# The first products of the MLP moved into the attention's last pair, on one core

## What is computed

```
attention (4 x 8 heads, 576 positions, head size 64):
  scores = q @ k.T / 8
  scores below (row maximum - tau) are dropped; softmax; attn @ v
MLP:      x = attention's output, as [2304, 512]
  h = x @ w_in            # [2304, 2048]
  y = relu(h)**2 @ w_out  # [2304, 512]
experts:  logits = y @ w_gate, best of 8 experts for each token,
  out = gate * sigmoid(y @ w_output_gate)[expert] * (relu(y @ w1[e]) @ w2[e])
```

## Time and profile before

| | us |
|---|---|
| median of 3 runs | 1022.42 |
| lowest and highest | 1020.78, 1023.05 |
| profiled execution, its own time | 1021.32 |
| span of its profile | 1019.6 |
| mean granted TensorE clock | 0.998 |

### The profile page before, as it was taken

The page is one execution under the profiler, slowest core; times in us unless marked ns, Lnnn a source line. Parts: engine busy times, 40 slices in busy tenths (PEclk is TensorE's granted clock), DMA queues, the critical chain, the costliest instruction groups (busy, mean ns, idle before and its releaser), DMA issues.

```text
span 1019.6 us, 19281 instructions
## 1 busy us (share of the span) xinstructions
PE 994.8 (98%) x6731; PEld 828.7 (81%) x6731; DVE 627.0 (61%) x1220; ACT 585.8 (57%) x922; POOL 418.3 (41%) x725
## 2 busy tenths in 40 slices
PE   7999999999998999999999999999999999999996
PEld 5888888888886888888888888889978888888884
DVE  5888888888885334322322232235787777777773
ACT  4888787787774333322322232233548888888883
POOL 4777778778783000000000000000008866666763
PEclk9999999999999999999999999999999999999999
DMA  4322322322213110010011001005389157351110
GB/s 115 80 61 71 86 55 71 87 61 69 59 30 95 42 52 1 21 42 21 1 42 42 0 21 42 22 1 161 124 328 401 49 196 283 116 197 41 34 41 34
DMA packets 85385, 84.04 MB, mean 82 GB/s; under 512 B 49711, under 2 KB 64559, under 8 KB 85298
## 3 DMA queue, kind: packets, MB, share of 16 engines
q1 hardware_dynamic: 81778, 72.41, 23.9%
q0 software_dynamic: 3520, 10.49, 3.0%
HBM read 69.24 MB, written 15.21 MB: 83 GB/s over the span
## 4 chain that ended last, share of the span: by engine, by line
PE 66%; DVE 1%; SPq 0%; issue 0%; ACT 0%; DMA 0%; POOL 0%; ACTq 0%; POOLq 0%; DVEq 0%
PE y_ps L1167 19%; PE h_ps L1150 19%; PE y_ps L1231 16%; PE row_ps L1231 8%; PE h_ps L1262 2%; PE row_ps L1136 2%; PE y_ps L1221 1%; SPq L969 0%; SPq L965 0%; DMA y_rows<-r_buf 0%; DVE g_lo L1488 0%; ACT r_buf L1335 0%; PE h_ps L1136 0%; POOL out_dram L1058 0%; DVE y_row L1701 0%
## 5 line engine op out<-in xcount | busy, mean ns | idle before, releaser
L1483 DVE TENSOR_TENSOR g_buf<-r_buf 128x512 f32<-128x512 f32 (+1 forms) x80 | 51.1, 638 | 220.5 <-ACT r_buf L1335 219.8
L1335 ACT ACTIVATE r_buf<-h_ps 128x512 f32<-128x512 f32 (+1 forms) x80 | 44.4, 555 | 234.1 <-PE h_ps L1150 231.9
L951 POOL TENSOR_TENSOR w_lo<-w_experts,w_hi 128x2048 fp32r<-128x2048 f32 x20 | 126.2, 6309 | 73.9 <-ACT w_hi L1394 73.7
L1394 ACT ACTIVATE w_hi<-w_experts 128x2048 fp32r (+1 forms) x100 | 150.4, 1564 | 0.5 <-PE row_ps L1231 0.5
L1069 POOL MEMSET ones<- 128x128 bf16 x1 | 0.2, 210 | 356.9 <-DVE x_lo L1469 356.9
L477 ACT ACTIVATE e_sb<-s_sb,stats,live 128x576 f32<-128x576 f32 x144 | 124.5, 865 | 37.8 <-POOL stats L265 36.5
L951 DVE TENSOR_TENSOR w_lo<-w_experts,w_hi 128x1024 fp32r<-128x1024 f32 (+1 forms) x80 | 137.0, 1754 | 5.3 <-ACT w_hi L1394 5.0
L1150 PE MATMUL h_ps<-x_hi,w_in_hi 128*128 128x512 f32 (+1 forms) x320 | 119.9, 375 | 2.3 <-DVE x_lo L1469 2.3
L1167 PE MATMUL y_ps<-g_hi,w_out_hi 128*128 128x512 f32 (+1 forms) x320 | 118.0, 369 | 0.9 <-DVE g_lo L1488 0.9
L1150 PE MATMUL h_ps<-x_hi,w_in_lo 128*128 128x512 f32 (+1 forms) x320 | 117.9, 368 | 0.0
L1150 PE MATMUL h_ps<-x_lo,w_in_hi 128*128 128x512 f32 (+1 forms) x320 | 117.8, 368 | 0.0
(11 more groups left out here) (251 smaller groups left out, 2217.8 us busy)
## 6 DMA issues: line engine op xcount, KB each, us to landing
w_experts<-in_moe_w_dram SPq DMA_DIRECT2D x18, 2048.0 KB, 13.9
y_rows<-y_row SPq DMA_DIRECT2D x36, 128.0 KB, 2.4
k_raw<-in_k_dram SPq DMA_DIRECT2D x32, 128.0 KB, 3.1
q_raw<-in_q_dram SPq DMA_DIRECT2D x32, 128.0 KB, 2.9
w_raw<-in_moe_w_in_dram SPq DMA_DIRECT2D x16, 256.0 KB, 3.2
v_nat<-in_v_dram SPq DMA_DIRECT2D x16, 256.0 KB, 2.6
y_T<-in_moe_w_out_dram SPq DMA_DIRECT2D x16, 256.0 KB, 2.7
y_early<-y_row SPq DMA_DIRECT2D x32, 128.0 KB, 2.4
```

The costliest lines, as they stand in the source:

```text
L951: alu.tensor_tensor(group_of(w_lo, g)[:, c0:c1], raw_group(buf, g)[:, c0:c1], group_of(w_hi, g)[:, c0:c1].bitcast(F32), ALU.subtract).then ...
L1394: nc.scalar.activation(group_of(w_hi, g)[:, c0:c1], raw_group(buf, g)[:, c0:c1], ACT.Copy).then_inc(hi_done, 1)
L1483: V.tensor_tensor(g_buf[:, 0:cols], r_buf[:, 0:cols], r_buf[:, 0:cols], ALU.mult).then_inc(sq_done, 1)
```

## The change

It does five things.

1. `x_hi`, `x_lo` and `y_T` get fixed places at the top of SBUF (`con[...]`), and the attention's buffers of the even pairs are allocated last, so that they lie in part under these. `h_ps`, the PSUM tile of the hidden products, is now allocated for both blocks, and the attention uses it as `s_ps[0]`.
2. Splitting the first 512 tokens of x moves into the attention: `first_x_hi(kc)` is the last thing that ACT does in steps 0 to 3 of pair 15, `first_x_lo(kc)` the last thing that DVE does in steps 1 to 4. They write into the places of the even pairs' buffers, so the first waits for the scores of pair 14.
3. The first four w_out loads are issued by SP in the attention once pair 14 is done, and so is the row of zeros, now from `w_raw`, with its memset on POOL ahead of the last `add_eps`. The relu's wait for the zeros is gone; SP waits for them ahead of the end of the block.
4. `first_hidden()`: PE makes the 12 matmuls of `hidden_group(0, 0)` at the end of the attention's block, behind `output_tail(15)`, and waits for their end.
5. In `moe`, `hidden_group(0, 0)` only counts up its semaphore; `split_x_group(0)`, the first loads and the memset are gone.

```diff
 @block.sync (attention), behind the loop over pairs
+            sp.wait_ge(tail_set, PAIRS - 1)
+            for n in range(4):
+                sp.dma_start(w_out_raw[:, n, :], w_out[n * P:(n + 1) * P, :]).then_inc(w_out_in, 16)
+            sp.wait_ge(zero_set, 1)
+            sp.dma_start(y_rows[DUMMY:DUMMY + 1, :], w_raw[0:1, :]).then_inc(zero_out, 16)
+            sp.wait_ge(w_out_in, 64)
+            sp.wait_ge(zero_out, 16)
 @block.gpsimd (attention), at the end
+            pool.wait_ge(w_split, 2 * LAST * PAIRS)
+            V.memset(w_raw[0:1, :], 0.0).then_inc(zero_set, 1)
             add_eps(PAIRS - 1)
 @block.tensor (attention), called behind the loop over steps
+            def first_hidden():
+                pe.wait_ge(xh_done, KC)
+                pe.wait_ge(max_done, CHUNKS * PAIRS)
+                for part, (w, x) in enumerate(((con["w_in_hi"], x_hi), (con["w_in_lo"], x_hi), (con["w_in_hi"], x_lo))):
+                    if part == 2:
+                        pe.wait_ge(xl_done, KC)
+                    for kc in range(KC):
+                        last = pe.matmul(s_ps[0][:, 0, :], w[:, 0, kc, :], x[:, kc * GROUP_T:(kc + 1) * GROUP_T],
+                                         start=(part == 0 and kc == 0), stop=(part == 2 and kc == KC - 1))
+                last.then_inc(hidden_made, 1)
+                pe.wait_ge(hidden_made, 1)
 @block.scalar (attention)
+            def first_x_hi(kc):
+                act.wait_ge(x_main_done, KC)
+                act.wait_ge(scores_ready, CHUNKS * (PAIRS - 1))
+                nc.scalar.activation(x_hi[:, kc * GROUP_T:(kc + 1) * GROUP_T], x_T[:, kc, 0:GROUP_T], ACT.Copy).then_inc(xh_done, 1)
                 if i < PAIRS and len(heads_in(c)) == 2:
                     exponential(i, c, 1)
+                if i == PAIRS - 1 and c < KC:
+                    first_x_hi(c)
 @block.vector (attention)
+            def first_x_lo(kc):
+                dve.wait_ge(xh_done, kc + 1)
+                V.tensor_tensor(x_lo[:, kc * GROUP_T:(kc + 1) * GROUP_T], x_T[:, kc, 0:GROUP_T],
+                                x_hi[:, kc * GROUP_T:(kc + 1) * GROUP_T].bitcast(F32), ALU.subtract).then_inc(xl_done, 1)
                 if c == 3 and i + 1 < PAIRS:
                     ends_lo(i + 1)
+                if i == PAIRS - 1 and 1 <= c <= KC:
+                    first_x_lo(c - 1)
 @block.sync (moe)
-            for n in range(4):
-                sp.dma_start(y_T[:, n, :], w_out[n * P:(n + 1) * P, :]).then_inc(w_raw_in[n], 16)
...
-            sp.wait_ge(zero_set, 1)
-            sp.dma_start(y_rows[DUMMY:DUMMY + 1, :], r_buf[0:1, :]).then_inc(zero_out, 16)
-            sp.wait_ge(zero_out, 16)
 @block.gpsimd (moe)
-            nc.gpsimd.memset(r_buf[0:1, :], 0.0).then_inc(zero_set, 1)
 @block.tensor (moe), hidden_group
+                if n == 0:
+                    pe.sem_inc(h_done, 1)
+                    return
 @block.scalar (moe)
             def split_w_out(f):
-                act.wait_ge(w_raw_in[f % 4], 16 * (f // 4 + 1))
+                if f >= 4:
+                    act.wait_ge(w_raw_in[f % 4], 16 * (f // 4))
...
-                if n == 0:
-                    act.wait_ge(zero_out, 16)
-                else:
+                if n >= 1:
                     act.wait_ge(sq_done, n)
                     act.wait_ge(g_hi_done, n)
...
-            split_x_group(0)
 @block.vector (moe)
-            split_x_group(0)
```

More of the change, by code:

```diff
@@ L98, in sets_in, with attention @@
     return 3 if c < LAST else 2
-def attention(nc, q, k, v, tau, w_in, con):
+def attention(nc, q, k, v, tau, w_in, w_out, y_rows, con):
     ident, x_T = con["ident"], con["x_T"]
+    x_hi, x_lo, w_out_raw = con["x_hi"], con["x_lo"], con["y_T"]
     qf = q.rearrange("b h s d -> (b h) s d")
@@ L116, in sem @@
             return ctx.enter_context(nc.semaphore(name))
-        q_raw = [sb(f"q_raw{b}", [P, QC, P]) for b in range(2)]
-        k_raw = [sb(f"k_raw{b}", [P, QC, P]) for b in range(2)]
-        v_nat = [sb(f"v_nat{b}", [P, 2, QC, D]) for b in range(2)]
+        q_raw, k_raw, v_nat = [None, sb("q_raw1", [P, QC, P])], [None, sb("k_raw1", [P, QC, P])], [None, sb("v_nat1", [P, 2, QC, D])]
         v_odd = [sb(f"v_odd{b}", [P, LAST, D]) for b in range(2)]
         v_mix = [sb(f"v_mix{b}", [P, P]) for b in range(2)]
-        qT_hi, qT_lo = ([sb(f"{n}{b}", [P, QC * P], F32R) for b in range(2)] for n in ("qT_hi", "qT_lo"))
-        kT_hi, kT_lo = ([sb(f"{n}{b}", [P, S], F32R) for b in range(2)] for n in ("kT_hi", "kT_lo"))
+        qT_hi, qT_lo = ([None, sb(f"{n}1", [P, QC * P], F32R)] for n in ("qT_hi", "qT_lo"))
+        kT_hi, kT_lo = ([None, sb(f"{n}1", [P, S], F32R)] for n in ("kT_hi", "kT_lo"))
         s_sb = [[sb(f"s_sb{b}{h}", [P, S]) for h in range(2)] for b in range(2)]
@@ L143, in attention @@
         w_raw = sb("w_raw", [P, WPART])
-        s_ps = [psum(f"s_ps{p}", [P, 2, 512]) for p in range(2)]
+        kept_to = nc.sbuf_base
+        v_nat[0] = sb("v_nat0", [P, 2, QC, D])
+        kT_hi[0], kT_lo[0] = (sb(f"{n}0", [P, S], F32R) for n in ("kT_hi", "kT_lo"))
+        qT_hi[0], qT_lo[0] = (sb(f"{n}0", [P, QC * P], F32R) for n in ("qT_hi", "qT_lo"))
+        q_raw[0], k_raw[0] = sb("q_raw0", [P, QC, P]), sb("k_raw0", [P, QC, P])
+        assert kept_to <= con["y_T_at"]
+        s_ps = [con["h_ps"], psum("s_ps1", [P, 2, 512])]
         t_ps = [psum(f"t_ps{p}", [P, 512]) for p in range(2)]
@@ L179, in attention @@
         x_tail_done = sem("x_tail_done")
+        w_out_in = sem("w_out_in")
+        hidden_made = sem("hidden_made")
+        zero_set, zero_out = sem("zero_row_set"), sem("zero_out")
+        xh_done, xl_done = sem("first_xh_done"), sem("first_xl_done")
         WPIECE = WPART // LAST
@@ L456, in _ @@
                     scores(*divmod(step + 1, STEPS))
+            first_hidden()
         @block.scalar
@@ L701, in moe @@
         w_out_lo = sb("w_out_lo", [P, FC, DM], F32R)
[L702 to L705, removed]
+        x_hi, x_hi_at, x_lo, x_lo_at = con["x_hi"], con["x_hi_at"], con["x_lo"], con["x_lo_at"]
         r_at = nc.sbuf_base
@@ L713, in moe @@
         g_lo = sb("g_lo", [P, 2 * GROUP_T], F32R)
-        y_T_at = nc.sbuf_base
-        y_T = sb("y_T", [P, KC, GROUP_T], F32)
+        y_T, y_T_at = con["y_T"], con["y_T_at"]
         y_row = con["y_row"]
         marks = sb("marks", [P, KC // 2, P + 4 * E], F32)
+        assert nc.sbuf_base <= y_T_at
         def region(at, size):
@@ L780, in moe @@
         factor_parts = on_g_top("factor_parts", [P, COLS, 3], BF16)
-        h_ps = psum("h_ps", [P, 2, 512])
+        h_ps = con["h_ps"]
         y_ps = [psum(f"y_ps{d}", [P, 512]) for d in range(KC)]
@@ L880, in split_before @@
         def split_before(q, kc):
-            return sum(KC * len(pieces(p)) for p in range(q)) + kc * len(pieces(q))
+            return sum(KC * len(pieces(p)) for p in range(1, q)) + kc * len(pieces(q))
         X_READ = split_before(ENDQ, KC)
@@ L1144, in hidden_group @@
                 for kc in range(KC):
-                    if f == 0:
+                    if f == 0 and q >= 1:
                         pe.wait_ge(xh_done, split_before(q, kc + 1))
@@ L1789, in program @@
         con["free_at"] = nc.sbuf_base
-        attention(nc, q, k, v, tau, w_in, con)
+        con["h_ps"] = keep.enter_context(nc.psum_tensor("h_ps", [P, 2, 512], F32))
+        top = nc.sbuf_top
+        for name, shape, dt in (("x_lo", [P, KC * GROUP_T], F32R), ("x_hi", [P, KC * GROUP_T], F32R),
+                                ("y_T", [P, KC, GROUP_T], F32)):
+            top -= 4 * KC * GROUP_T
+            con[name + "_at"] = top
+            con[name] = nc.alloc_sbuf_tensor_at(name, shape, dt, offset=top)
+        attention(nc, q, k, v, tau, w_in, w_out, y_rows, con)
         moe(nc, w_out, w_gate, w_output_gate, w1, w2, y_rows, y_early, out, con)
```

2 lines of the change are left out of this document (removed).

## The result

| | us |
|---|---|
| changed kernel, median of 5 runs | 1030.03 (1028.38 to 1031.66) |
| kernel before, median of 5 runs | 1021.59 (1020.78 to 1023.05) |
| ratio, 95% interval | 1.0077 (1.0065 to 1.0088) |
| profiled execution after: span | 1028.2 (before 1019.6) |

The forecast was 1020.9 with a range of 1019.0 to 1022.5. The page of the changed kernel looks like the page of before, but for one number: PE has the same 6731 matmuls and is busy 9.5 us longer.

The account below looks back on a forecast made before the run. PE, busy 98% of the span, was taken as the bound. A 2.6 us gain at the border less 1.1 for held POOL gave -1.5 us on the profiled 1021.32; against the runs' median the forecast was 1020.9, range 1019.0 to 1022.5.

Parts of the forecast that it names:

- The rest of the kernel shifts as a whole: Beyond the border, MLP and experts keep their pace, as PE is the bound and its progress releases all loads.
- The border: Between attention and MLP, the first output product comes at 323.1 instead of 325.69, a gain of 2.6 us.
- my bound of 2.3: Lowest gain at the border, if PE's wait for its last matmul and the step cost twice 0.31 us.
- The holds: In pair 15, DVE's x_lo subtractions stop POOL's small operations; attention ends 1.1 us later, bounds 0 and 2.8.
- ACT's four copies, the DMAs and the memset: In the attention's end, covered by idle time and so free; uncovered, copies 0.55 us each, memset half a us.
- If the granted clock at the border falls from 1.00, all of part 1 is wrong: Sign set for the border: a clock below 1.00 there would refute its gain and the whole forecast.
- part 1: The gain between attention and MLP from earlier first products, x split and relu: 2.6 us, bounds 2.3 and 3.2.
- C: Rival: DVE becomes the last pair's bound, attention ends 3.7 us later, 1.1 slower in sum, 1023.5; chance 0.06.
- the mark that I had set for it: Sign for the rival of DVE as bound: output_tail ends past 319.6, where the forecast had near 318.2.

Follow-up runs that it names:

- e2: Changed kernel with x_hi, x_lo and y_T 1408 bytes lower, aligned with the other operands as before the change: 1022.13 us, ratio 0.9995.
- e1: Kernel before with only x_hi, x_lo and y_T at the changed kernel's addresses, no work moved: 1030.19 us, ratio 1.0069.
- e5: e4 without first_hidden, so the first 12 products stay in the MLP's block: 1018.46 us, ratio 0.9971.
- e3: Changed kernel with the four x_lo subtractions behind the last reciprocal, in DVE's idle time: 1027.37 us, ratio 1.0043.
- e4: Changed kernel with the three tiles 1408 bytes lower and the x_lo subtractions in DVE's idle time: 1018.85 us, ratio 0.996.
- s2: e4 with x_hi, x_lo, y_T and marks 128 bytes higher: 1027.18 us, a single run.
- s4: e3 with the tiles 128 bytes lower, 1280 bytes off the other operands: 1018.69 us, a single run.
- s1: e4 with x_hi, x_lo, y_T and marks 32 bytes higher: 1029.24 us, a single run.
- s5: e4 with x_hi, x_lo, y_T and marks 64 bytes higher: 1027.84 us, a single run.
- f1: e4 with POOL's last w_in split moved behind the biases and cuts of the last step: 1017.45 us, ratio 0.996.

## Why the prediction was wrong

1. **The step that failed: "The rest of the kernel shifts as a whole".** Item 1 of the change, the new addresses, got no price at all, not even bounds; I read it as what made room for the rest. In its place the runs show that both the MLP and the experts run slower, 232.8 ns for a hidden product instead of 227.4, because three tiles lie 1408 bytes off: 7.9 us (changed kernel to e2, and e1 to the kernel before). No row of before prices a distance directly, but there may have been a trace in it: the hidden products behind the rows at L1136 are slower than others on the same code. A question of it ("why do equal matmuls differ?") would have shown that the pace depends on more than columns and clock.

The Trainium skill would not have warned (page "SBUF — State Buffer", section "Who interferes with whom"): it has PE never waiting on anyone at SBUF. That rule is on one engine against another; the runs show a price without another engine, 227.4 against 232.8 ns by nothing but the distance between PE's own two operands, and the measurement decides.

2. **The border (right in kind, 2.6 forecast, 2.05 found).** The chain was as described: the relu starts right behind its w_out copy (323.90), and its two halves are there at 326.05, 0.35 ahead of PE's own 326.40. The sum is below my bound of 2.3, since PE's pause between the blocks was 0.73, longer than the twice 0.31 that this bound allowed.

3. **The holds (right in kind, 1.1 forecast, 1.66 found for the `biases` of the last step).** I followed POOL's queue up to the second mask and overlooked that x_lo(3) stands on DVE right behind it, so that the same instruction is held twice: 311.04 instead of 310.5. The two instructions at 298.34 and 306.20 show the same, 1.31 and 1.39 for a mask and an x_lo behind it. The last mask was late by 1.66 (312.27 for 310.61), where I had 1.5.

4. **ACT's four copies, the DMAs and the memset cost nothing**, as forecast: e5 has all of them, and its `output_tail` ends at 317.05, for 317.06 before. In the changed kernel the w_out loads are issued from 301.41, and POOL's memset lies at 312.12, ahead of the last `add_eps`.

5. **The clock.** "If the granted clock at the border falls from 1.00, all of part 1 is wrong": it fell, for 3.4 us ahead of the border, and cost 1.1 us in this profile; the gain of part 1 came nonetheless, as the fall was over when the tail ended. e1 has a fall with the gaps of before. e3 and e4 have one with a gap of 1.63 to 1.64 in the last pair, and s2, s4 and e5 have none with the same gap. So it doesn't follow from the length of the gap alone. It goes with the scatter of one kernel's runs: of those of the kernel before beside e1 to e4, four at a mean clock of 0.993 take 1023.0 to 1023.5 and two at 0.998 take 1021.2 and 1021.3. It is no part of the 8, which s1, s2 and s5 show without a fall.

6. **The rivals.** None had the mechanism. C, slower through DVE, was the closest in sign, and the mark that I had set for it was met: `output_tail` ended past 319.6, at 319.82. But 1.1 us of that are the clock, and PE's gap of 2.44 ends behind an exponential that had waited 2.37 us for POOL's `biases`, not for DVE.

Without the addresses (e2) the time would have been in the stated range, 1022.13 for 1020.9. Of the error of 9.1 us, 7.9 are the term that was not in the sum. For the other 1.2 the holds and the border, mis-sized by some 0.6 each, would be enough; the clock's share differs from run to run. That e2 lies so near the kernel before doesn't bear out the 1.1 and the 2.6: both were off.

## What to carry to other kernels

Where a change moves a tile that a matmul reads, price the address too: for float32r products of 512 columns like these, keep the distance between the stationary and the moving operand at a multiple of 256 bytes within the partition, and check by the number of matmuls in a stretch in which PE is fully busy at full clock. A DVE instruction with two SBUF inputs put beside POOL's small operations costs what it delays there, not what it takes on DVE, and one queued right behind another holds the same POOL instruction twice. When the last pair of a pipeline hangs on a queue of tiny operations, moving one piece of bulk work behind them (f1) gave 1.0 to 1.4 us, and moving the next stage's first products ahead gave nothing (e5). What the border gave came from splitting x ahead of it and from the relu's wait that is gone; no run parts these two.

## What the hardware showed that I had not expected

- Matmuls of 512 float32r columns at 2.4 GHz run at 226.7 to 228 ns on the mean if the two operands are a multiple of 256 bytes apart, and at 230.0 to 233.3 ns on the mean (single hidden products 224 to 238) if they are 32, 64, 128 or 1408 bytes apart. It shows at once and is gone some three to ten matmuls after the last such pair. Products of 256 columns don't show it (118.9 against 120.4 ns).
- TensorE was at half clock for 3.4 or 6.8 us around the border, where it pauses for 1.6 to 2.4 us, in 6 of the 14 profiled executions, and stayed at full clock with the same pauses in others (e1 against the kernel before). What decides stays open.
- POOL's 128x1 operation that meets two two-input DVE instructions in a row took 1.33 us; its shortest is 0.285.
